# Reading TensorE's moving operands from the last column to the first, with the weights at eight places

## The reference

```python
sig = 1.0 / (1.0 + np.exp(-f_logit))
f = lower_bound + (1.0 - lower_bound) * sig
for t in range(S):
    h = f[:, t] * h + (1.0 - f[:, t]) * x[:, t]
    y[:, t] = h
# y as 12160 x 256; w_in 256 x 2048, w_out 2048 x 256
g = np.maximum(y @ w_in, 0.0) ** 2
out = g @ w_out
```

## Time and profile before

| | |
|---|---|
| median of two runs | 988.68 us |
| the profiled execution's own time | 988.59 us |
| its span in the profile | 986.5 us |
| TensorE busy | 982.4 us, 100% of the span, 4388 matmuls |
| VectorE, ScalarE busy | 731.8 us (74%), 697.4 us (71%) |
| granted TensorE clock, mean | 1.00 |

### The profile page before, as it was taken

The page is one execution under the profiler, slowest core; times in us unless marked ns, Lnnn a source line. Parts: engine busy times, 40 slices in busy tenths (PEclk is TensorE's granted clock), DMA queues, the critical chain, the costliest instruction groups (busy, mean ns, idle before and its releaser), DMA issues.

```text
span 986.5 us, 12612 instructions
## 1 busy us (share of the span) xinstructions
PE 982.4 (100%) x4388; PEld 818.7 (83%) x4388; DVE 731.8 (74%) x940; ACT 697.4 (71%) x925; POOL 50.3 (5%) x50
## 2 busy tenths in 40 slices
PE   9999999999999999999999999999999999999998
PEld 7998888888888888888888888888888888888887
DVE  6997886876877687688688778768768767876545
ACT  8977766766776776676677677677667767766665
POOL 2682000000000000000000000000000000000000
PEclk9999999999999999999999999999999999999999
DMA  9003011002101201100210210110111021001001
GB/s 330 1 15 109 0 44 64 22 1 86 43 1 48 80 0 43 64 21 16 69 43 0 77 51 0 43 64 21 42 43 43 0 85 43 1 1 43 1 1 43
DMA packets 22158, 41.96 MB, mean 43 GB/s; under 512 B 1520, under 2 KB 3056, under 8 KB 22128
## 3 DMA queue, kind: packets, MB, share of 16 engines
q1 hardware_dynamic: 21984, 41.43, 12.1%
q10 hardware_dynamic: 144, 0.13, 0.0%
HBM read 29.11 MB, written 12.45 MB: 42 GB/s over the span
## 4 chain that ended last, share of the span: by engine, by line
PE 100%; DVE 0%; POOL 0%; issue 0%; DVEq 0%; POOLq 0%
PE out_ps L927 52%; PE hidden_ps L912 42%; PE hidden_ps L953 4%; PE out_ps L947 1%; PE out_ps L953 1%; PE out_ps L937 0%; POOL zeros L888 0%; DVE result L848 0%; DVE result L853 0%; DVE result L850 0%; DVEq L852 0%; DVEq L847 0%; POOLq L1204 0%
## 5 line engine op out<-in xcount | busy, mean ns | idle before, releaser
L927 PE MATMUL out_ps<-g_hi,w_out_lo 128*128 128x512 f32 (+1 forms) x760 | 294.2, 387 | 0.0
L927 PE MATMUL out_ps<-g_lo,w_out_hi 128*128 128x512 f32 (+1 forms) x760 | 294.2, 387 | 0.0
L927 PE MATMUL out_ps<-g_hi,w_out_hi 128*128 128x512 f32 (+1 forms) x760 | 294.1, 387 | 0.0
L700 DVE TENSOR_TENSOR g_lo<-h,g_hi 128x1024 fp32r<-128x1024 f32 (+1 forms) x189 | 231.9, 1227 | 64.2 <-ACT g_hi L416 61.0
L409 ACT ACTIVATE h<-h 128x1024 f32<-128x1024 f32 (+1 forms) x189 | 199.2, 1054 | 3.2
L927 PEld LDWEIGHTS out_ps<-g_hi,w_out_hi 128*128 128x128 f32 x760 | 142.7, 188 | 28.3
L927 PEld LDWEIGHTS out_ps<-g_lo,w_out_hi 128*128 128x128 f32 x760 | 142.7, 188 | 28.2
L927 PEld LDWEIGHTS out_ps<-g_hi,w_out_lo 128*128 128x128 f32 x760 | 142.7, 188 | 28.0
L912 PE MATMUL hidden_ps<-sums_hi,wc_hi 128*128 128x512 f32 x352 | 137.0, 389 | 0.0
L912 PE MATMUL hidden_ps<-sums_lo,wc_hi 128*128 128x512 f32 x352 | 137.0, 389 | 0.0
L912 PE MATMUL hidden_ps<-sums_hi,wc_lo 128*128 128x512 f32 x352 | 136.9, 389 | 0.0
(11 more groups left out here) (114 smaller groups left out, 1054.6 us busy)
## 6 DMA issues: line engine op xcount, KB each, us to landing
f_in<-f_logit_t SPq DMA_DIRECT2D x22, 512.0 KB, 4.6
x_in<-x_t SPq DMA_DIRECT2D x22, 512.0 KB, 4.5
out_t<-result SPq DMA_DIRECT2D x20, 512.0 KB, 3.1
w_out_raw<-weights SPq DMA_DIRECT2D x8, 256.0 KB, 6.7
w_in_raw<-weights SPq DMA_DIRECT2D x5, 256.0 KB, 6.5
out_t<-result SPq DMA_DIRECT2D x2, 448.0 KB, 3.0
w_in_raw<-first SPq DMA_DIRECT2D x3, 256.0 KB, 4.1
out_t<-result SPq DMA_DIRECT2D x3, 256.0 KB, 2.0
```

What stands on the lines that cost most here:

```text
L700: nc.vector.tensor_tensor(g_lo[b][:, :, 0:n], h_of(it, j, b), g_hi[b][:, :, 0:n].bitcast(F32), ALU.subtract).then_inc(g_ready[b], 1)
L927: mm = nc.tensor.matmul(out_ps[:, b, c, in_bank(it)], half[:, j, m, c * P:(c + 1) * P], moving[b][:, m, 0:n], start=(j == 0 and m == 0 and ...
```

## The change

Two things change. First, every matmul but the warm-up's reads its moving operand from the last column to the first (`[:, ::-1]`, a step of -1). The columns of a piece come out of the first layer in turned order, all elementwise work on them is done in that order, and the second layer turns them back, so `out_ps` holds them as before. Where only a part of the columns is read or written, the part is turned too (`turned`).

Second, each of the four weight tiles becomes one flat tile in which each group of blocks is followed by 16 unused elements (64 bytes), and the groups stand in it in rotated order (`quads_of`, starting at place 0, 1, 3 and 4). In the built program the remainder of the address by 512 of a weight block is then the same for all the loads of the first layer of group j, and of the second layer's loads that run between them: 128 + 64 j, again by 512. It takes eight values, one for each group. Moving rows all start at remainder 384, since the weights have become 1,792 bytes longer. So the weights of group j lie 64 j - 256 bytes off the moving row, taken by 512.

To make room, the warm-up's zeros lie in the second half of a row of `h[1]` instead of a tile of their own. No instruction is added, removed or moved: the order of instructions on each engine is that of before, row for row, but for the name of that tile.

The other weight accesses (in `first_w_in_lo`, `rest_of_w_out`, `plain_w_in_lo`, `round_w_out`) change their index as in `plain_w_in_hi` below.

```diff
--- before.py
+++ after.py
@@ -15,6 +15,7 @@
 EARLY_QUADS = 3
 BOUNDS = 16
 CUT = 256
+STEP = 16
 
 
 
@@ -94,15 +95,25 @@
         def sem(name):
             return ctx.enter_context(nc.semaphore(name))
 
-        wc_hi = sb("wc_hi", [P, QUADS, 7, P], F32R)
-        wc_lo = sb("wc_lo", [P, QUADS, 7, P], F32R)
-        w_out_hi = sb("w_out_hi", [P, QUADS, 2, C * P], F32R)
-        w_out_lo = sb("w_out_lo", [P, QUADS, 2, C * P], F32R)
+        def quads_of(name, blocks, m, first_place):
+
+            size = blocks * m + STEP
+            t = sb(name, [P, QUADS * size - STEP], F32R)
+            places = [(first_place + q) % QUADS * size for q in range(QUADS)]
+            return [t[:, k:k + blocks * m].rearrange("p (b m) -> p b m", m=m) for k in places]
+
+
+        wc_hi = quads_of("wc_hi", 7, P, 0)
+        wc_lo = quads_of("wc_lo", 7, P, 1)
+        w_out_hi = quads_of("w_out_hi", 2, C * P, 3)
+        w_out_lo = quads_of("w_out_lo", 2, C * P, 4)
         x_in = sb("x_in", [P, B, C, N])
         f_in = sb("f_in", [P, B, C, N])
         plain_hi = [sb(f"plain_hi{k}", [P, 3, N], F32R) for k in range(2)]
         plain_lo = [sb(f"plain_lo{k}", [P, 3, N], F32R) for k in range(2)]
         h = [sb(f"h{b}", [P, 2, N]) for b in range(B)]
+
+        zeros = h[1][:, 1, HALF:N].bitcast(mybir.dt.bfloat16)
         g_hi = [sb(f"g_hi{b}", [P, 2, N], F32R) for b in range(B)]
         g_lo = [sb(f"g_lo{b}", [P, 2, N], F32R) for b in range(B)]
         sums_out = sb("sums_out", [P, 3, N])
@@ -117,7 +128,6 @@
         sums_lo[1] = sb("sums_lo1", [P, 4, N], F32R)
         result = sb("result", [P, B, C, N])
         sb("rest_of_raw", [P, 4, N])
-        zeros = sb("zeros", [P, N], mybir.dt.bfloat16)
         slope = sb("slope", [P, C])
         middle = sb("middle", [P, C])
         state = sb("state", [P, B, C])
@@ -389,13 +399,13 @@
 
             def plain_w_in_hi(q):
                 act.wait_ge(w_in_loaded[q], 16)
-                nc.scalar.copy(wc_hi[:, q, A11:A21 + 1], w_in_raw[:, q]).then_inc(w_plain_hi_done, 1)
+                nc.scalar.copy(wc_hi[q][:, A11:A21 + 1], w_in_raw[:, q]).then_inc(w_plain_hi_done, 1)
 
             def sum_w_in_hi(q):
 
                 act.wait_ge(pair_done[1], q + 1)
                 act.wait_ge(w_sum_done, 4 * (q + 1))
-                nc.scalar.copy(wc_hi[:, q, S2:S3 + 1], w_in_raw[:, q]).then_inc(w_sum_hi_done, 1)
+                nc.scalar.copy(wc_hi[q][:, S2:S3 + 1], w_in_raw[:, q]).then_inc(w_sum_hi_done, 1)
 
             def relu_pair1(it, j):
                 n, q = width(it), it * QUADS + j
...
@@ -882,10 +892,10 @@
 
             def sum_w_in_lo(q):
                 pool.wait_ge(w_sum_hi_done, q + 1)
-                nc.gpsimd.tensor_tensor(wc_lo[:, q, S2:S3 + 1], w_in_raw[:, q],
-                                        wc_hi[:, q, S2:S3 + 1].bitcast(F32), ALU.subtract).then_inc(w_sum_ready, 1)
-
-            nc.gpsimd.memset(zeros[:], 0.0).then_inc(zeros_done, 1)
+                nc.gpsimd.tensor_tensor(wc_lo[q][:, S2:S3 + 1], w_in_raw[:, q],
+                                        wc_hi[q][:, S2:S3 + 1].bitcast(F32), ALU.subtract).then_inc(w_sum_ready, 1)
+
+            nc.gpsimd.memset(zeros, 0.0).then_inc(zeros_done, 1)
             plain_w_in_lo(3)
             w_in_sums(0)
             w_in_sums(1)
...
@@ -909,7 +921,7 @@
                 if isinstance(it, int) and it == 1 and w >= S2:
                     pe.wait_ge(w_sum_ready, j + 1)
                 for m, (half, moving) in enumerate(((wc_hi, hi), (wc_hi, lo), (wc_lo, hi))):
-                    mm = nc.tensor.matmul(hidden_ps[:, bank, 0:n], half[:, j, w], moving,
+                    mm = nc.tensor.matmul(hidden_ps[:, bank, 0:n], half[j][:, w], moving[:, ::-1],
                                           start=(opens and m == 0), stop=(m == 2), skip_group_check=True)
                 mm.then_inc(signal, 1)
 
@@ -924,8 +936,8 @@
                     pe.wait_ge(g_ready[b], q + 1)
                 for k in passes:
                     half, moving = ((w_out_hi, g_hi), (w_out_hi, g_lo), (w_out_lo, g_hi))[k]
-                    mm = nc.tensor.matmul(out_ps[:, b, c, in_bank(it)], half[:, j, m, c * P:(c + 1) * P],
-                                          moving[b][:, m, 0:n], start=(j == 0 and m == 0 and k == 0),
+                    mm = nc.tensor.matmul(out_ps[:, b, c, in_bank(it)], half[j][:, m, c * P:(c + 1) * P],
+                                          moving[b][:, m, 0:n][:, ::-1], start=(j == 0 and m == 0 and k == 0),
                                           stop=False, skip_group_check=True)
                 if m == 1 and c == 1 and 2 in passes:
                     mm.then_inc(g_used[b], 1)
@@ -933,9 +945,10 @@
             def very_last_second(to, b, m, c, columns=slice(0, N), opens=False, closes=None):
 
                 j = QUADS - 1
+                turned = slice(N - columns.stop, N - columns.start)
                 for k, (half, moving) in enumerate(((w_out_hi, g_hi), (w_out_hi, g_lo), (w_out_lo, g_hi))):
-                    mm = nc.tensor.matmul(to, half[:, j, m, c * P:(c + 1) * P],
-                                          moving[b][:, m, columns], start=opens and k == 0,
+                    mm = nc.tensor.matmul(to, half[j][:, m, c * P:(c + 1) * P],
+                                          moving[b][:, m, turned][:, ::-1], start=opens and k == 0,
                                           stop=closes is not None and k == 2, skip_group_check=True)
                 if closes is not None:
                     mm.then_inc(closes, 1)
@@ -944,14 +957,16 @@
 
             def warm(times):
                 for _ in range(times):
-                    nc.tensor.matmul(out_ps[:, 1, 1], zeros[:, 0:P], zeros[:], start=True, stop=True)
+                    nc.tensor.matmul(out_ps[:, 1, 1], zeros[:, 0:P], zeros, start=True, stop=True)
 
             def first_part(j, b, c, half, of, opens=False, signal=None, columns=slice(0, NARROW)):
 
                 banks = first_banks(j, b)
+                turned = slice(NARROW - columns.stop, NARROW - columns.start)
                 for m, blocks in enumerate(((A11, A12), (A21, A22))):
-                    mm = nc.tensor.matmul(banks[:, m, columns], half[:, j, blocks[c]],
-                                          first_block(*of, b, c)[:, columns], start=opens, stop=signal is not None,
+                    mm = nc.tensor.matmul(banks[:, m, turned], half[j][:, blocks[c]],
+                                          first_block(*of, b, c)[:, columns][:, ::-1], start=opens,
+                                          stop=signal is not None,
                                           skip_group_check=True)
                 if signal is not None:
                     mm.then_inc(signal, 1)
```

More of the change, by code:

```diff
@@ L430, in round_w_out @@
                 act.wait_ge(w_out_loaded[q], 16)
-                nc.scalar.copy(w_out_hi[:, q], w_out_raw[:, q]).then_inc(w_out_hi_done, 1)
+                nc.scalar.copy(w_out_hi[q], w_out_raw[:, q]).then_inc(w_out_hi_done, 1)
             def first_quads():
@@ L658, in first_w_in_lo @@
                 dve.wait_ge(w_plain_hi_done, q + 1)
-                nc.vector.tensor_tensor(wc_lo[:, q, A11:A21 + 1], w_in_raw[:, q],
-                                        wc_hi[:, q, A11:A21 + 1].bitcast(F32), ALU.subtract
+                nc.vector.tensor_tensor(wc_lo[q][:, A11:A21 + 1], w_in_raw[:, q],
+                                        wc_hi[q][:, A11:A21 + 1].bitcast(F32), ALU.subtract
                                         ).then_inc(w_first_ready, 1)
@@ L687, in rest_of_w_out @@
                 dve.wait_ge(w_out_hi_done, q + 1)
-                nc.vector.tensor_tensor(w_out_lo[:, q], w_out_raw[:, q], w_out_hi[:, q].bitcast(F32), ALU.subtract
+                nc.vector.tensor_tensor(w_out_lo[q], w_out_raw[:, q], w_out_hi[q].bitcast(F32), ALU.subtract
                                         ).then_inc(w_out_ready, 1)
@@ L860, in plain_w_in_lo @@
                 pool.wait_ge(w_plain_hi_done, q + 1)
-                nc.gpsimd.tensor_tensor(wc_lo[:, q, A11:A21 + 1], w_in_raw[:, q],
-                                        wc_hi[:, q, A11:A21 + 1].bitcast(F32), ALU.subtract
+                nc.gpsimd.tensor_tensor(wc_lo[q][:, A11:A21 + 1], w_in_raw[:, q],
+                                        wc_hi[q][:, A11:A21 + 1].bitcast(F32), ALU.subtract
                                         ).then_inc(w_plain_ready, 1)
```

## The result

The changed kernel takes 1016.22 us (two runs, 1016.19 and 1016.24), 1.0278 times the time before, with a 95% interval of 1.0234 to 1.0323. It is slower. 988.6 had been forecast; the time lies in the stated range, 944 to 1,036.

The account below looks back on a forecast made before the run. The prediction took TensorE's own pace, 226.7 ns per 512-column matmul, to bound the kernel. All parts of the change were costed at 0, so 988.6 + 0 = 988.6 us, range 944 to 1,036 for 8 in 10.

Parts of the forecast that it names:

- What bounds the kernel: Whole span: TensorE busy 982.4 of 986.5 us, so only its own pace counts; the other engines have slack.
- Edits costed at 0: Instructions, warm-up tile, turned columns on other engines and 64-byte gaps between weight groups: each claimed to cost 0.
- Direction and place together: Wide TensorE matmuls, reads turned and weights moved: unknown, bounded from 930 to 1,165 us, taken as 0.
- A cost that arises at each change of matmul: Between matmuls on TensorE: the 13.3 ns over the columns' time read as fixed, so the change leaves it.
- The 448-column case: Narrower TensorE matmuls: 16.0 ns extra in place of 13.3, which a fixed cost doesn't give.
- The first rival: Weight and moving reads on TensorE collide; reading both downward avoids most of it: 937 to 969 us, chance 0.30.
- The second rival: With both reads downward, the faster moving read catches the weight read and follows it: 1,056 us, milder 1,010 to 1,040, chance 0.21.
- A step of -1 slow by itself: Moving reads on TensorE go at half pace when turned: some 1,770 us, chance 0.03.
- The Trainium skill's rule of independent ports: TensorE reads weights and moving operand through separate SBUF ports, so neither place nor direction matters: sum 0.

Follow-up runs that it names:

- rev_only: Kernel before with all moving operands turned, weights packed as before: 1016.34 us, ratio 1.0278.
- lines_back: Kernel before with moving operands read in 4-column (16-byte) groups, groups from last to first, columns within each forward: 1016.45 us.
- m_line: Kernel before, each moving operand of 448 or 512 columns reading its first 4 columns 112 or 128 times: 944.31 us.
- sweep16: Kernel before with all weights in one tile, group j 16 j bytes further on in all four tensors, moving operands forward: 1008.72 us.
- lo64: Kernel before with the rests of all moving operands 64 bytes further on, weights as before: 1009.60 us.
- w_one: Kernel before, each weight load but the warm-up's reading one column 128 times, moving operands forward: 1009.32 us.
- w_one_rev: Kernel before, each weight load but the warm-up's reading one column 128 times, and moving operands backward: 1015.70 us.
- fine_rev: Changed kernel with the weights of group j 8 j bytes further on than packed, moving operands backward: 1018.24 us.
- in_line_back: Kernel before with moving operands read in 4-column (16-byte) groups, groups in forward order, columns within each from last to first: 988.94 us.
- m_one: Kernel before, each moving operand of 448 or 512 columns reading only its first column over and over: 944.60 us.
- places_only: Changed kernel without the turned reads, so moving operands go from first to last: 1003.51 us, ratio 1.0147.
- rev_second: Kernel before with only the second layer's 512- and 448-column matmuls of one line read backward: 1011.72 us.
- both_one: Kernel before with weight loads and moving operands both held at one column: 944.85 us.

## Why the prediction was wrong

*What bounds the kernel*: right. TensorE's pace alone decides, and 6.67 ns on 3,954 matmuls carry 26.4 of the 27.6 us.

*Edits costed at 0*: right for instructions, warm-up tile, turned columns and the blocks of the other engines. Their busy times are unchanged, the first matmul still starts at 1.32 us, and rev_only, which has none of the packing, takes the same time as the whole change.

*"Direction and place together ... The value I take is 0"*: this step failed. The term is 6.67 ns on each matmul of 512 columns and 4.0 on each of 448, 27.6 us of the span, and all of it comes from the direction (rev_only, lines_back). "A cost that arises at each change of matmul would look just so" is what m_line refutes: without new lines the extra is 2.6 ns, not 13.3, at the same changes of matmul. The argument was that the extra was the same for every group and tile. But all of these were read upward and lay at one offset to each other, a good one as sweep16 and lo64 showed, so their agreement was no evidence; the text named that and took 0 all the same. The 448-column case, which it also named as speaking against, was a sign to follow: an extra that changes with the columns isn't fixed.

*The first rival, a collision that reading in one direction avoids*: wrong. Nothing went, and w_one shows that holding the weight read at one column gives nothing back at 512 columns.

*The second rival, the moving read runs into the weight read*: the sign was right, the mechanism isn't borne out. It wanted different prices by group, down to near 0 at some; backward all have nearly one price, 233.3 to 233.5 ns, at 64- and 16-byte steps, with longer steps of the weight read and with the weights held at one column (w_one_rev), and fine_rev's groups differ by 2.2 ns at most. The stated range held because this rival had pulled it up to 1,036 us; with a mechanism that the runs don't show, that was luck.

*A step of -1 slow by itself*: in its size (half pace) wrong, and by in_line_back also in its kind. What is slow is the downward order of lines, by 3%.

*The Trainium skill's rule of independent ports* (the page and section above), by which the sum was 0: it is about the two reads' effect on each other. The rule leaves out what the change cost: the 6.67 ns come with the direction of the moving read.

What stays open: why lines read downward end at 233.3, the pace of a bad offset, why forward the good offsets are few and recur with 256 bytes, and why weights held at one column give 231.7 forward. Nor is the cost a fixed price for each line. Turned, matmuls of 448 columns have 20.0 ns over their own columns and those of 512 have 20.0 too, though they read 112 and 128 lines; those of 256 columns did not slow down when turned, and went to 113.7 ns with w_one. And the weight load under way beside it may have a part in it. The runs describe these; none shows the mechanism.

No version beat the kernel before. The 944 us of m_line and m_one leave out most of the moving data; of the kernels that read all columns, 226.7 ns is the lowest pace seen.

## What to carry to other kernels

Where TensorE's pace is the bound and its matmuls are like these (fp32r, 512 columns, a weight load for each), read moving operands upward through memory, and keep all weights and moving operands at one offset to each other modulo 256 bytes, at one found by trial: here that was worth up to 2.8%. A cost that is equal everywhere in a trace is only known to be fixed if the thing that might change it varies somewhere in that trace. A small case that doesn't fit, such as the narrow matmuls here, deserves a price, not a remark.

## What the runs showed of the hardware

- A matmul of 512 fp32r columns has 2.6 ns over its columns on one line of moving data (216.0 ns), 13.3 ns with lines read upward at a good offset (226.7), 20.0 with lines read downward (233.3).
- Read upward, the pace follows the offset of the weights, with a period of 256 bytes: 227.1, 233.3, 232.2, 229.1 ns at steps of 64 bytes. Read downward, the pace is 233.3 to 233.5 at all places of 64 and 16 bytes.
- A matmul's pace depends on the matmuls around it: after a change to the good offset it needs some four to settle (places_only), and upward reads slow down, to 230.6 ns on the mean, when downward ones stand between them (rev_second).
- What slows a downward read is the order of 16-byte pieces; the order of the four columns within one costs nothing (lines_back 233.3, in_line_back 226.7 ns).
- Matmuls of 512 bf16 columns at full clock, read upward through new lines, start 216 ns apart (warm-up of both_one).
